# Chunked mLSTM followed by two feed-forward layers on one core: the state update moved ahead of the denominators, matmuls of ones added in the late units, and three steps of the later stages moved

## Chip, cores and metric

One core of one Trainium2 chip. The metric is the device time of one execution in microseconds (us), lower is better. The time before is the median of three runs; a profiled execution is told apart from them below.

## What is computed

Three layers, one after the other. B, H, S, D are 2, 8, 768, 40; the model width is H*D = 320 and there are 1536 tokens.

```python
# 1: per token t, state C (D x D) and n (D) of each head
m_new = max(f[t] + m, i[t]); f_stab = exp(f[t] + m - m_new); i_stab = exp(i[t] - m_new)
C = f_stab * C + i_stab * outer(v[t], k[t]);  n = f_stab * n + i_stab * k[t]
y[t] = sigmoid(o[t]) * (C @ q[t]) / max(abs(n . q[t]), 1)
# 2: four experts, all of them for every token
x = sum over e of p[:, e] * (relu(x @ w1[e]) @ w2[e])        # w1: 320 x 1024, w2: 1024 x 320
# 3: gated layer
out = ((x @ w_a) * (x @ w_b)) @ w_out                         # 320 x 1536, 1536 x 320
```

## The kernel before

**First layer, in units.** The sequence is cut into chunks of 128 tokens; a unit is one chunk of one batch, so there are NU = 12 units, and batch b of unit u is u % 2. For each unit TensorE (PE) makes the scores of queries and keys (`products`, L1245), the products with the incoming state (`from_state`, L1257), the products of weighted scores and values (`outputs`, L1286) and the addition to the state (`update`, L1271); `log_weights` (L1233, L1234) makes the decay weights of the next unit. The order on PE is written out by hand: in the loop over u come `log_weights(u + 1)`, `products(u)`, `from_state(u)`, in units 3 to 8 the turning of an earlier unit's finished output (`x_transpose`, four transposes, L1202 and L1204), `outputs(u - 1)` and `update(u - 1)`. `from_state(u)` waits for the state that `add_update(u - 2)` leaves.

VectorE (DVE) multiplies scores by weights (`weigh`, L896), scales the products with the state (`scale_inter`, L904), takes the numerators (`take_num`, L932), divides (`normalise`: three small instructions for the denominators, L940 to L944, and one for the quotient, L948), and adds to the state (`add_update`, L921), in this order. GpSimd (POOL) decays the state (L428), gates the output (`gate_output`, L441) and does parts of the weights: `sums` are four additions of 128 x 128 (L457 to L463), `low_a` and `low_s` the low halves of a split of the float32 weights in two (L447, L452). ScalarE (ACT) makes the high halves (`high_a` L633, `high_s` L637) and copies.

**Second and third layers, in groups.** The rest of the program is NG = 56 groups, of which the first FIRST = 32 belong to the experts and the others to the gated layer. A group makes two blocks of 128 hidden columns for half of the tokens by a scheme of seven products of half-size blocks instead of eight (`product(n, i)`, four matmuls each, L1358 to L1361, into two PSUM banks A and B in turn), and between them, in slots, the second layer of the group before (`second_layer`, L1382). How many of its matmuls go into each slot is the table `chunks(n)`. ACT copies three of the products out (`keep_p1` L675, `keep_u2` L681, `keep_w` L687); DVE adds to them (`make_c11` L1056, `make_c22` L1063, `make_c12` L1070) and makes the low halves of the hidden values (`low_relu` L1041, `low_product` L1047). Product 5 waits for `keep_w`, product 6 for `make_c22`, and the first product of the next group for the low half of the second hidden block (`a_free`).

The input of these groups is itself held as seven sums and differences of blocks: `x_sum` (four subtractions, on DVE L880 or on POOL L489), `x_high` (ACT L597) and `x_low` (DVE L870, L871). There are four such sets of input, numbered s = 0 to 3. Sets 1, 2 and 3 are turned by PE within groups 1 and 2, 29 and 30, 33 and 34 (`turning(n)`): three turns (`turn_within`) in each of these groups, each into bank B, each copied out by ACT (`keep_turn`, L582) before the bank is written again. `set_at(n, k)` is the set that stands k steps after its base in group n; so the x_sums of set 1 lie in groups 2 and 3, those of set 2 in groups 30 and 31, and in groups 4, 32 and 36 the products of a new set begin.

`keep_busy` (L1211) and `keep_warm` (L1217) are matmuls of constants whose results nobody reads; there are 32 of ones in units 0 and 1 and 13 of the identity in group 0.

Of the kernel before, what the change touches and what calls it, by code (L numbers as in the profile page):

```python
# [53 lines left out]
def mlstm_moe_kernel(nc, qk_t, tok, gates, late, probs, wt, wtail, w2, w_out, out):  # L54
    with ExitStack() as ctx:
# [156 lines left out]
            return 4 * min(n, FIRST) + 2 * max(n - FIRST, 0)  # L212

        BASES = {1: 0, 2: FIRST - NP1, 3: FIRST}
        TURN_AFTER = (0, 1, 2)

        def set_at(n, k):

# [34 lines left out]
        def chunks(n):  # L253

            if turning(n) is not None:
                return (3, 6, 5, 0, 3, 6, 1, 5, 4, 3) if n <= FIRST else (0, 3, 3, 0, 2, 3, 0, 3, 2, 2)
            if n == NG - 1:
                return (0, 2, 1, 1, 3, 3, 8)
            return (4, 5, 5, 5, 8, 5, 4) if n <= FIRST else (0, 3, 2, 2, 5, 4, 2)
# [130 lines left out]
        def _(pool):  # L390
# [101 lines left out]
            for u in range(NU):  # L492
                if B <= u < OLD:
                    decay_state(u)
                if u < OLD:
                    update_keys(u)
                if u >= 1:
                    sigmoid(u - 1)
                    gate_output(u - 1)
                if u == 3:  # L500
                    tails_low_a(0)
                if u == 4:
                    tails_sums(0)
                if u == 5:
                    tails_low_s(0)
                    low_a(0)
                if u == 6:
                    sums(0)
                if u == 7:
                    low_s(0)  # L510
                    low_a(1)
                if u == 8:
                    sums(1)
                if u in (8, 9, 10):
                    x_sum(0, u - 8)
                if u == 10:
                    x_sum(0, 3)
            sigmoid(NU - 1)
            low_s(1)
            gate_output(NU - 1)  # L520
            for i in range(2, NP1):
                low_a(i)
                sums(i)
# [1 line left out]
            for n in range(NG):  # L525
                st = n // (2 * NP1)
                if set_at(n, 3) == 3:
                    for j in range(1, 4):
                        x_sum(3, j)
                for i in range(NP1, NS * NP1):  # L530
                    if a_at(i) + 1 == n:
                        low_s(i)
                    if a_at(i) == n:
                        low_a(i)
                        sums(i)
                if n % (2 * NP1) == 4 and st + 1 < NS:
                    tails_low_a(st + 1)
                    tails_sums(st + 1)
                if n % (2 * NP1) == 5 and st + 1 < NS:
                    tails_low_s(st + 1)  # L540
                if set_at(n, 2) == 3:
                    x_sum(3, 0)


        @block.scalar
        def _(act):
# [174 lines left out]
            for u in range(1, NU):  # L721
                if u == 1:
                    gates_of(1)
                if u + 1 < NU:
                    weights(u + 1)
                if u == 1:
                    act.wait_ge(ex_turned, 2)
                    nc.scalar.activation(ex[:, :, :, :].rearrange("p a c h -> p (a c h)"), PS[:, XPOSE, BH:BH + 3 * REST], ACT.Exp).then_inc(ex_ready, 1)
                if u >= 2:
                    replicate((u - 2) // UB, (u - 2) % UB)  # L730
                if 0 <= u - 3 < UB:
                    keep_turned(0, u - 3, XPOSE)
                if u >= 2:
                    gates_of(u)
                if u == 2:
                    nc.scalar.dma_start(t1[:, :], wtail[0, :, :]).then_inc(t1_in, 16)
                if 2 <= u <= NP1 + 1:
                    load_first(u - 2)
                if 6 <= u <= 9:
                    load_first_w2(u - 6)  # L740
                if u == 3:
                    tails_high_a(0)
                if u == 4:
                    high_a(0)
                if u == 5:
                    tails_high_s(0)
                if u == 6:
                    high_a(1)
                if u == 7:
                    high_s(0)  # L750
                if u == 9:
                    high_s(1)
                if 6 <= u <= 10:
                    x_high(0, u - 6)
                if u in (9, 10):
                    high_w2(u - 9)
                if u == 11:
                    x_high(0, 5)
                    x_high(0, 6)
# [26 lines left out]
            def expert_group(n):  # L786
# [8 lines left out]
                if b2 is not None:  # L795
                    x_high(b2, 0)
                high_c11(n)
                keep_turn(n, 1)
                keep_u2(n)
                keep_turn(n, 2)  # L800
                if b2 is not None:
                    x_high(b2, 1)
                if b3 is not None:
                    x_high(b3, 3)
                prepare_weights(n)
                keep_w(n)
                replicate_late(b1, 3)
                if b2 is not None:
                    x_high(b2, 2)
# [11 lines left out]
            def gated_group(n):  # L821
# [11 lines left out]
                    high_product(n - 1, 1)  # L833
                if b2 is not None:
                    x_high(b2, 0)
                keep_turn(n, 1)
                keep_u2(n)
                keep_turn(n, 2)
                if b2 is not None:
                    x_high(b2, 1)  # L840
                if b3 is not None:
                    x_high(b3, 4)
                keep_w(n)
                replicate_late(b1, 3)
                if b2 is not None:
                    x_high(b2, 2)
                prepare_weights(n)
                if b3 is not None:
                    x_high(b3, 5)
# [13 lines left out]
        def _(dve):  # L863
# [158 lines left out]
            for u in range(NU):  # L1022
                if u == 0:
                    rest_logs()
                weigh(u)
                if u >= B:
                    scale_inter(u)
                if u >= 1:
                    take_num(u - 1)
                    normalise(u - 1)  # L1030
                    if u - 1 < OLD:
                        add_update(u - 1)
                if u >= 7:
                    x_low(0, u - 7)
                if u == 11:
                    low_w2(0)
# [73 lines left out]
            def expert_group(n):  # L1110
# [16 lines left out]
                if b3 is not None:  # L1127
                    x_low(b3, 3)
                    x_sum(b3, 1)
                    x_sum(b3, 2)  # L1130
                if b4 is not None:
                    x_low(b4, 5)
                    x_low(b4, 6)
                make_c22(n)
                if p == 0:
                    add_tiles(n, range(HB))
                w2_lows(n)
                low_relu(n, 1, PS[:, A_BANK, 0:HT])
                low_relu(n, 2, c22_s[:, :])
# [7 lines left out]
                    x_low(b2, 2)  # L1147
                    x_sum(b2, 0)
                if b3 is not None:
                    x_sum(b3, 3)  # L1150
                    x_low(b3, 4)

            def gated_group(n):
# [40 lines left out]
        def _(pe):  # L1194
# [228 lines left out]
            for u in range(1, NU):  # L1423
# [3 lines left out]
                if u == 1:  # L1427
                    keep_busy(3)
                    log_weights(2)
                if u >= B:  # L1430
                    from_state(u)
                if 0 <= u - 3 < UB:
# [6 lines left out]
            for n in range(NG):  # L1439
                slot = 0  # L1440
                for i in range(7):
                    product(n, i)
                    between(n, slot)
                    slot += 1
                    if turning(n) is not None and i in TURN_AFTER:
                        turn_within(n, TURN_AFTER.index(i))
                        between(n, slot)
                        slot += 1
            for j in range(3 * HB * tiles(NG - 1)):
# [37 lines left out]
```

## Time and profile before

| | us |
|---|---|
| median of three runs | 637.74 |
| lowest, highest | 635.42, 637.91 |
| the profiled execution | 639.25 |
| its span, first to last instruction | 637.5 |
| PE busy | 617.9 (97%) |
| VectorE, ScalarE, GpSimd busy | 374.3, 301.6, 217.1 |
| mean granted TensorE clock | 0.977 |

The units take the first 87.7 us of the span, group 0 the next 15.1, and the groups after it the rest. A float32 matmul of the units shows as two instructions in the trace. "Busy" of PE is from a matmul's start to its modelled end, so that a busy PE can still be at half its clock; the granted clock is a row of its own. The waits view puts idle time of an engine down to the instruction that ended it.

### The profile page before, as it was taken

Reading aid. Unit: us, or ns where it says so; the run is one execution under the profiler, and the core shown is the slowest. Engines: PE = TensorE matmul, PEld = TensorE weight load, DVE = VectorE, ACT = ScalarE, POOL = GpSimd, SP = SyncE. Lnnn points to the kernel's source line nnn. Section 1 sums busy time; section 2 is a strip of 40 time slices with the busy share of each in tenths; the row PEclk is TensorE's granted clock in tenths of the full one; section 3 lists DMA queues with packets and bytes.
Section 4 is the critical chain, followed back from the end, with each engine's and each line's share of the span. In section 5 each row is a group of like instructions: output and inputs, shape, how many; then the busy total and the mean of one; then the engine's idle time right before and its main releaser. Section 6 shows DMA issues by size and latency. Waiting matters only on the chain. (4 is left out here: it accounts for less than half of the span.)

```text
span 637.5 us, 11103 instructions
## 1 busy us (share of the span) xinstructions
PE 617.9 (97%) x4005; PEld 594.1 (93%) x4015; DVE 374.3 (59%) x716; ACT 301.6 (47%) x644; POOL 217.1 (34%) x285
## 2 busy tenths in 40 slices
PE   8999999999999999999999999998989999999997
PEld 7888798989999999999999999988879999999997
DVE  6667785676354444463534635377597564656565
ACT  3688734653444333543435434665554443444332
POOL 3378863304250033510243201254144640463000
PEclk9999659999999999999999999999999999999999
DMA  3657504100232002320014100112100420030011
GB/s 119 197 198 190 157 0 135 55 22 1 66 93 75 22 1 66 93 75 22 1 44 104 55 12 1 45 23 83 53 12 1 99 85 28 9 80 1 1 63 62
DMA packets 21062, 38.96 MB, mean 61 GB/s; under 512 B 3600, under 2 KB 11312, under 8 KB 21008
## 3 DMA queue, kind: packets, MB, share of 16 engines
q1 hardware_dynamic: 18976, 35.57, 19.8%
q10 hardware_dynamic: 2032, 2.68, 1.5%
q8 instruction: 32, 0.52, 0.3%
q14 instruction: 22, 0.18, 0.1%
HBM read 26.42 MB, written 1.97 MB: 45 GB/s over the span
## 5 line engine op out<-in xcount | busy, mean ns | idle before, releaser
L1382 PE MATMUL PS<-w2h,hh 128*128 128x320 f32 x528 | 164.3, 311 | 0.0
L1382 PE MATMUL PS<-w2h,hl 128*128 128x320 f32 x528 | 163.8, 310 | 0.0
L1382 PE MATMUL PS<-w2l,hh 128*128 128x320 f32 x528 | 163.3, 309 | 0.0
L1358 PE MATMUL PS<-xop,wop 128*128 128x384 f32 x392 | 139.9, 357 | 9.4 <-DVE c_s L1063 2.3
L669 ACT ACTIVATE hh<-c_s 128x384 fp32r<-128x384 f32 x144 | 75.3, 523 | 130.7 <-DVE c_s L1070 42.2
L1361 PE MATMUL PS<-xop,wop 96*128 96x384 f32 x392 | 132.9, 339 | 0.0
L1359 PE MATMUL PS<-xop,wop 128*128 128x384 f32 x392 | 132.6, 338 | 0.0
L1360 PE MATMUL PS<-xop,wop 128*128 128x384 f32 x392 | 132.5, 338 | 0.0
L1063 DVE TENSOR_TENSOR c_s<-PS,w_s 128x384 f32<-128x384 f32 x56 | 31.2, 557 | 124.1 <-ACT w_s L687 89.1
L1382 PEld LDWEIGHTS PS<-w2h,hh 128*128 128x128 f32 x528 | 99.6, 189 | 0.8 <-DVE hl L1047 0.7
L1382 PEld LDWEIGHTS PS<-w2l,hh 128*128 128x128 f32 x528 | 99.6, 189 | 0.0
L1382 PEld LDWEIGHTS PS<-w2h,hl 128*128 128x128 f32 x528 | 99.5, 188 | 0.0
L1358 PEld LDWEIGHTS PS<-xop,wop 128*128 128x128 f32 x392 | 74.1, 189 | 19.8 <-issue 4.0
L452 POOL TENSOR_TENSOR wop<-s,wop 128x512 fp32r<-128x512 f32 x28 | 37.2, 1327 | 136.4 <-ACT wop L637 136.4
L1041 DVE SCALAR_TENSOR_TENSOR hl<-c_s,hh 128x384 fp32r<-128x384 f32 x96 | 55.0, 572 | 41.9 <-ACT hh L669 41.7
L1359 PEld LDWEIGHTS PS<-xop,wop 128*128 128x128 f32 x392 | 74.3, 190 | 0.0
L1361 PEld LDWEIGHTS PS<-xop,wop 96*128 96x128 f32 x392 | 74.1, 189 | 0.0
L1360 PEld LDWEIGHTS PS<-xop,wop 128*128 128x128 f32 x392 | 74.1, 189 | 0.0
L687 ACT ACTIVATE w_s<-PS 128x384 f32<-128x384 f32 x56 | 27.5, 490 | 75.3 <-PE PS L1361 75.2
L471 POOL TENSOR_TENSOR t1l<-t,t1h 128x384 fp32r<-128x384 f32 x7 | 7.1, 1020 | 130.2 <-ACT t1h L643 130.2
L1056 DVE TENSOR_TENSOR c_s<-PS,p_s 128x384 f32<-128x384 f32 x56 | 31.0, 554 | 21.6 <-PE PS L1361 21.3
L447 POOL TENSOR_TENSOR wop<-s,wop 128x384 fp32r<-128x384 f32 x28 | 29.8, 1065 | 40.7 <-ACT wop L633 40.7
(137 smaller groups left out, 867.6 us busy)
## 6 DMA issues: line engine op xcount, KB each, us to landing
wop<-t1h SPq DMA_DIRECT2D x56, 112.0 KB, 2.2
s<-in_wt SPq DMA_DIRECT2D x24, 256.0 KB, 3.2
kvo<-in_tok SPq DMA_DIRECT2D x12, 480.0 KB, 4.3
qk<-in_qk_t SPq DMA_DIRECT2D x24, 160.0 KB
s<-in_w SPq DMA_DIRECT2D x12, 320.0 KB, 3.0
wop<-t1l SPq DMA_DIRECT2D x28, 112.0 KB, 2.2
s<-in_w_out SPq DMA_DIRECT2D x12, 160.0 KB, 2.2
out_y<-acc SPq DMA_DIRECT2D x12, 160.0 KB, 1.9
```

The costliest lines, as they stand in the source:

```text
L447: nc.gpsimd.tensor_tensor(wop[p][:, 2, 0:3 * P], s1[:, p, P:4 * P], f32(wop[p][:, 0, 0:3 * P]), ALU.subtract).then_inc(w_lo_a, 1)
L452: nc.gpsimd.tensor_tensor(wop[p][:, 2, 3 * P:7 * P], s1[:, p, :], f32(wop[p][:, 0, 3 * P:7 * P]), ALU.subtract).then_inc(w_lo_s, 1)
L669: nc.scalar.activation(hh[:, home(n, k), :], src, ACT.Relu if n < FIRST else ACT.Copy).then_inc(hh_ready, 1)
L687: nc.scalar.activation(w_s[:, :], PS[:, A_BANK, 0:HT], ACT.Copy).then_inc(w_kept, 1)
L1041: nc.vector.scalar_tensor_tensor(out=hl[:, home(n, k), :], in0=src, scalar=0.0, in1=f32(hh[:, home(n, k), :]), op0=ALU.max, op1=ALU.subtra ...
L1056: nc.vector.tensor_tensor(c11_s[:, :], PS[:, B_BANK, 0:HT], p1_s[:, :], ALU.add).then_inc(c11_made, 1)
L1063: nc.vector.tensor_tensor(c22_s[:, :], PS[:, B_BANK, 0:HT], w_s[:, :], ALU.add).then_inc(c22_made, 1)
L1358: nc.tensor.matmul(bank, ws[0], xs[0], start=opens, stop=False, skip_group_check=True)
L1359: nc.tensor.matmul(bank, ws[0], xs[2], start=False, stop=False, skip_group_check=True)
L1360: nc.tensor.matmul(bank, ws[2], xs[0], start=False, stop=False, skip_group_check=True)
L1361: nc.tensor.matmul(bank, ws[1][0:96, :], xs[1][0:96, :], start=False, stop=closes, skip_group_check=True).then_inc(prod_done, 1)
L1382: got = nc.tensor.matmul(bank, left, (w2l if part == 1 else w2h)[p][:, f, :], start=opens and part == 0, stop=closes and part == 2)
```

## The change

In the units, `add_update(u - 1)` stands ahead of `normalise(u - 1)` on DVE. In units 7 to 11 PE does three matmuls of ones between `products(u)` and `from_state(u)`, behind a wait for `scale_inter(u - 1)`, since they write into the same bank that it reads. The four additions `sums(1)` on POOL move from unit 8 to behind the units, ahead of the last `gate_output`; `high_s(1)` on ACT moves from unit 9 to group 0, ahead of `keep_w`, and the other weights that ACT prepares in group 0 move behind `keep_w`. In the turning groups the second and third turn stand behind the third product, instead of behind the second and the third, with other counts in the slots and with `keep_u2` ahead of the second copy. The third x_sum of sets 1 and 2 moves behind `make_c22`, their fourth from DVE to POOL. In group 35 `x_high` of step 4 moves behind `keep_w`.

```diff
-        TURN_AFTER = (0, 1, 2)
+        TURNS_AFTER = {0: (0,), 2: (1, 2)}
...
             if turning(n) is not None:
-                return (3, 6, 5, 0, 3, 6, 1, 5, 4, 3) if n <= FIRST else (0, 3, 3, 0, 2, 3, 0, 3, 2, 2)
+                return (3, 6, 1, 0, 6, 6, 1, 6, 4, 3) if n <= FIRST else (0, 5, 1, 0, 4, 4, 0, 3, 1, 0)
...
# POOL, units
-                if u == 8:
-                    sums(1)
...
             sigmoid(NU - 1)
+            sums(1)
+            gate_output(NU - 1)
             low_s(1)
-            gate_output(NU - 1)
...
# POOL, groups
+                if set_at(n, 3) in (1, 2):
+                    x_sum(set_at(n, 3), 3)
...
# ACT, units
-                if u == 9:
-                    high_s(1)
...
# ACT, expert_group
+                keep_u2(n)
                 keep_turn(n, 1)
-                keep_u2(n)
                 keep_turn(n, 2)
...
-                prepare_weights(n)
+                if n:
+                    prepare_weights(n)
+                else:
+                    high_s(1)
                 keep_w(n)
+                if n == 0:
+                    prepare_weights(n)
...
# ACT, gated_group
-                if b3 is not None:
-                    x_high(b3, 4)
                 keep_w(n)
                 replicate_late(b1, 3)
                 if b2 is not None:
                     x_high(b2, 2)
+                if b3 is not None:
+                    x_high(b3, 4)
...
# DVE, units
                     take_num(u - 1)
-                    normalise(u - 1)
                     if u - 1 < OLD:
                         add_update(u - 1)
+                    normalise(u - 1)
...
# DVE, expert_group
                     x_sum(b3, 1)
-                    x_sum(b3, 2)
...
                 make_c22(n)
                 if p == 0:
                     add_tiles(n, range(HB))
+                if b3 is not None:
+                    x_sum(b3, 2)
...
-                    x_sum(b3, 3)
                     x_low(b3, 4)
...
# PE
+                if u > UB:
+                    pe.wait_ge(inter_scaled, u - B)
+                    keep_busy(3)
                 if u >= B:
                     from_state(u)
...
-                    if turning(n) is not None and i in TURN_AFTER:
-                        turn_within(n, TURN_AFTER.index(i))
+                    for k in TURNS_AFTER.get(i, ()) if turning(n) is not None else ():
+                        turn_within(n, k)
```

The instructions of PE in unit 9 (scores, state, outputs, addition to the state), before:

```order
L1245 MATMUL PS<-qk 128x128 x8
L1257 MATMUL PS<-state,qk 128x82 x4
L1286 MATMUL PS<-vx,pt 128x41 x8
L1271 MATMUL PS<-vx,kw 40x41 x8
L1233 MATMUL PS<-mask,identb 128x512
```

And with the change (every line number of PE is four higher):

```order
L1249 MATMUL PS<-qk 128x128 x8
L1215 MATMUL PS<-ones 128x128 x3
L1261 MATMUL PS<-state,qk 128x82 x4
L1290 MATMUL PS<-vx,pt 128x41 x8
L1275 MATMUL PS<-vx,kw 40x41 x8
L1237 MATMUL PS<-mask,identb 128x512
```

The three matmuls of ones stand where PE had only the wait for the state. In the same unit on DVE, from the scaling of the products with the state to the quotient, before:

```order
L904 TENSOR_TENSOR inter_s<-PS,ex 128x328
L932 TENSOR_TENSOR num<-PS,inter_s 128x328
L940 SCALAR_TENSOR_TENSOR den<-num 128x8
L942 TENSOR_SCALAR den<-den 128x8
L944 RECIPROCAL den<-den 128x8
L948 TENSOR_TENSOR normed<-num,den 128x320
L921 TENSOR_TENSOR state<-PS,state 40x4x41 x2
```

With the change:

```order
L908 TENSOR_TENSOR inter_s<-PS,ex 128x328
L936 TENSOR_TENSOR num<-PS,inter_s 128x328
L925 TENSOR_TENSOR state<-PS,state 40x4x41 x2
L944 SCALAR_TENSOR_TENSOR den<-num 128x8
L946 TENSOR_SCALAR den<-den 128x8
L948 RECIPROCAL den<-den 128x8
L952 TENSOR_TENSOR normed<-num,den 128x320
```

The two additions to the state now run before four instructions that they don't need, and the quotient behind two more than before. On ACT, from the end of the last unit into group 0, before:

```order
L597 ACTIVATE xop<-raw 128x2x384 x2
L675 ACTIVATE p_s<-PS 128x384
L669 ACTIVATE hh<-c_s 128x384
L681 ACTIVATE u_s<-PS 128x384
L633 ACTIVATE wop<-s 128x384
L687 ACTIVATE w_s<-PS 128x384
L669 ACTIVATE hh<-PS 128x384
```

With the change:

```order
L598 ACTIVATE xop<-raw 128x2x384 x2
L676 ACTIVATE p_s<-PS 128x384
L670 ACTIVATE hh<-c_s 128x384
L682 ACTIVATE u_s<-PS 128x384
L638 ACTIVATE wop<-s 128x512
L688 ACTIVATE w_s<-PS 128x384
L634 ACTIVATE wop<-s 128x384
L670 ACTIVATE hh<-PS 128x384
```

The copy of the fifth product (w_s) no longer stands behind the high half of a weight that waits for the last gated output, but behind one that waits for the four additions of `sums(1)`.

## Rows read from the trace of the kernel before

**Rows 1.** Page, parts 1 and 2: busy time, and the granted clock in 40 slices.

```profile
PE 617.9 (97%) x4005; PEld 594.1 (93%) x4015; DVE 374.3 (59%) x716; ACT 301.6 (47%) x644; POOL 217.1 (34%) x285
...
PEclk9999659999999999999999999999999999999999
```

**Rows 2.** Waits of PE: waiting <- waited for: us in total, times, longest.

```profile
PE PS L1257 <- DVE state L921: 2.4, 4, 1.0
...
PE PS L1358 <- DVE xop L871: 2.2, 4, 0.8
...
PE PS L1358 <- ACT w_s L687: 1.7, 2, 1.3
```

**Rows 3.** Windows of 2 us: length, busy of each engine, then clock, DMA, GB/s.

```profile
66.00:68.00 2.00, 1.23 (x11) 1.23 (x12) 1.91 (x5) 0.90 (x4) 1.72 (x3) 1.00 0.98 272
68.00:70.00 2.00, 2.00 (x17) 1.92 (x16) 1.90 (x4) 2.00 (x6) 1.84 (x4) 0.77 0.58 181
...
86.00:88.00 2.00, 2.00 (x10) 2.00 (x11) 0.11 (x2) 0.76 (x2) 2.00 (x3) 0.50 0.00 0
...
96.00:98.00 2.00, 2.00 (x14) 2.00 (x14) 1.76 (x6) 0.31 (x1) 0.00 (x0) 0.91 0.00 0
```

**Rows 4.** Timeline, PE: from_state of units 7 to 11, first product of group 0.

```profile
53.70 1.12 PE L1257 MATMUL PS<-state,qk 128*128 128x82 f32 x8 [0.59 <-DVE state L921]
...
59.94 1.12 PE L1257 MATMUL PS<-state,qk 128*128 128x82 f32 x8 [0.42 <-DVE state L921]
...
66.77 1.12 PE L1257 MATMUL PS<-state,qk 128*128 128x82 f32 x8 [1.02 <-DVE state L921]
...
74.54 2.00 PE L1257 MATMUL PS<-state,qk 128*128 128x82 f32 x8
...
82.53 2.00 PE L1257 MATMUL PS<-state,qk 128*128 128x82 f32 x8
...
87.67 0.67 PE L1358 MATMUL PS<-xop,wop 128*128 128x384 f32 x1
```

**Rows 5.** Timeline, DVE, unit 9: numerators, quotient, state.

```profile
63.83 0.49 DVE L932 TENSOR_TENSOR num<-PS,inter_s 128x328 f32<-128x328 f32 x1
...
65.63 0.49 DVE L948 TENSOR_TENSOR normed<-num,den 128x320 f32<-128x320 f32 x1
66.04 0.68 DVE L921 TENSOR_TENSOR state<-PS,state 40x164 f32<-40x164 f32 x2
```

**Rows 6.** Timeline, PE, unit 1: three matmuls of ones and the next.

```profile
17.82 0.94 PE L1211 MATMUL PS<-ones 128*128 128x128 f32 x6
18.59 0.38 PE L1233 MATMUL PS<-mask,identb 128*128 128x512 bf16 x1
```

**Rows 7.** Timeline, PE: sixth product of group 0, first of group 1.

```profile
100.53 0.41 PE L1358 MATMUL PS<-xop,wop 128*128 128x384 f32 x1 [1.25 <-ACT w_s L687]
...
102.81 0.42 PE L1358 MATMUL PS<-xop,wop 128*128 128x384 f32 x1
```

**Rows 8.** Timeline, PE: last product of group 3, third of group 4.

```profile
136.89 0.44 PE L1358 MATMUL PS<-xop,wop 128*128 128x384 f32 x1 [0.34 <-DVE c_s L1063]
...
141.63 0.44 PE L1358 MATMUL PS<-xop,wop 128*128 128x384 f32 x1 [0.46 <-DVE xop L871]
```

**Rows 9.** Timeline, groups 31 and 32.

```profile
426.95 3.62 DVE L880 TENSOR_TENSOR raw<-raw 128x768 f32<-128x768 f32 x2
...
431.09 0.44 PE L1358 MATMUL PS<-xop,wop 128*128 128x384 f32 x1 [1.92 <-DVE c_s L1063]
...
431.36 0.54 DVE L1041 SCALAR_TENSOR_TENSOR hl<-PS,hh 128x384 fp32r<-128x384 f32 x1
...
432.49 0.34 PE L1358 MATMUL PS<-xop,wop 128*128 128x384 f32 x1
...
435.96 0.44 PE L1358 MATMUL PS<-xop,wop 128*128 128x384 f32 x1 [0.59 <-DVE xop L871]
```

**Rows 10.** Timeline, PE, group 33: second product, second turn, fourth product.

```profile
445.51 0.44 PE L1358 MATMUL PS<-xop,wop 128*128 128x384 f32 x1 [0.24 <-ACT raw L582]
...
447.13 0.33 PE L1202 MATMUL PS<-identf,acc 128*128 128x128 f32 x1 [0.21 <-DVE c_s L1056]
...
450.01 0.41 PE L1358 MATMUL PS<-xop,wop 128*128 128x384 f32 x1 [0.33 <-ACT raw L582]
```

More of the change, by code:

```diff
@@ L835, in gated_group @@
                     x_high(b2, 0)
+                keep_u2(n)
                 keep_turn(n, 1)
-                keep_u2(n)
                 keep_turn(n, 2)
```

## The prediction

> **What bounds the kernel now.** I read the page first. PE is busy for 617.9 of 637.5 us, so only two things can give much: its clock and its few waits. The row of the clock shows both levels: 9 (2.4 GHz) nearly everywhere, but 6 and 5 in the fifth and sixth of the 40 slices, from 64 to 96 us [rows 1]. The windows of 2 us place it: 1.00 up to 68 us, 0.77 in the next (half of the clock from about 69.1 on), 0.50 until 96, and 0.91 in the window at 96, so full again from about 96.4 [rows 3]. That is 27.3 us at 1.2 GHz, and PE is busy without a break in nearly all of it: there each microsecond of work at the full clock takes two.
>
> The timeline says where this lies: `from_state` of unit 9 begins at 66.77, after PE had been idle for 1.02 us; units 10 and 11 follow at 74.54 and 82.53, and group 0 begins at 87.67 [rows 4]. What did PE do before the clock fell? Units 7 and 8 had idle times of 0.59 and 0.42 us and four transposes each, and held the clock; unit 9 is the first with the longer idle and without transposes. The idle time ends each time with DVE's addition to the state. On DVE, numerators begin at 63.83, quotient at 65.63, state at 66.04 [rows 5]: 1.7 us of denominators and quotient stand between, which the state does not need.
>
> The waits view lists the rest: 2.4 us for the state, 2.2 for low halves of the input (x_low), 1.7 for w_s, of which 1.3 in group 0 [rows 2]. I looked at each in the timeline [rows 7 to 10].
>
> **The change part by part.** The sum is made against the profiled execution, 639.25 us (span 637.5); the median of the runs, 637.74, is 1.5 below it, which I take off at the end.
>
> *State ahead of the denominators.* The state comes about 1.7 us earlier behind the numerators. The waits of units 7, 8 and 9 (0.59, 0.42, 1.02) go, and one of 0.36 in unit 6 (2.4 less these, [rows 2]). Late next is the quotient, by the 0.68 us of the additions: behind it are the gated output on POOL, ACT's copy of it and the values for the next outputs. They are wanted a unit later, so I cost that at nothing; without that cover it would be 0.7 us a unit.
>
> *Ones.* Three matmuls took 17.82 to 18.59 at the full clock, 0.77 us [rows 6]. There are five units with them. In units 7 and 8 they cost 1.54, and with unit 6 the waits give back 1.37: together +0.2.
>
> *Units 9 to 11 and group 0, if the clock holds.* Unit 8 to unit 9 took 6.83 us at the full clock [rows 4]; without the 1.02 and with ones that is 6.58: -0.25. From unit 9 to 10 the transposes are gone too (0.4 or so): 6.2 for 7.77, -1.6. From unit 10 to 11, where no decay weights are left to make, 7.99 at half clock is 4.0 at full, 4.8 with ones. DVE can't follow that: its work of a unit fills most of 1.91 and 1.90 in windows of 2 us beside POOL [rows 3], so some 6 us a unit. I take 5.8: -2.2; the bounds are 4.8 and 6.6. From there to group 0: 5.14, half is 2.6: -2.5. Group 0 took 102.81 - 87.67 = 15.14 us. Of it 8.7 ran at half clock (87.67 to 96.4), 4.4 at full; the other 6.4 contain the wait of 1.25 for w_s [rows 7], which `keep_w` ahead of the weights removes. That leaves 9.5. But now DVE and ACT are late: DVE has x_low, low_w2 and the last numerators ahead of c11, and w_s stands behind `high_s(1)`, which waits for POOL to finish the last x_sums, two sigmoids and `sums(1)`. I put 1.6 on it (bounds 0.5 and 3): 11.1, so -4.0. These four come to **-10.6** (bounds -8 and -12.5).
>
> The Trainium skill (TensorE: Matmul & The Clock Gate, Part 1 and "Why this matters for your kernels") says the clock follows how busy PE was, and advises against idle gaps between matmuls. The rows agree with the gap before the fall, but not that busy time alone gives the clock back: the window at 86 us is full of PE work at 0.50. By that rule alone the ones would still do, since they fill the gap.
>
> *Groups 3 and 4.* The last product of group 3 waited 0.34 for c22 behind two x_sums; the third of group 4 waited 0.46 for x_low [rows 8], behind the fourth. One x_sum now runs behind c22, one on POOL. With the restart of the pipeline after each wait, -1.0.
>
> *Groups 31 and 32.* The wait is larger, 1.92 us, since two x_sums took 3.62 us beside POOL's work [rows 9]. But it does not all come back: group 32's first product must wait for hl, at 431.36 + 0.54 = 431.90, and DVE has the same work ahead of that as before. So 432.49 becomes 431.95 at best: -0.5. The 0.59 at the third product of group 32 shrinks as the fourth x_sum leaves DVE, though POOL then works beside it: -0.2. Together -0.7 (bounds 0 and -1.2).
>
> The Trainium skill (SBUF — State Buffer, "Who interferes with whom") says that a DVE instruction with two inputs in SBUF contends with a reading GpSimd one. By it a subtraction on POOL is not free to DVE: with the whole of it charged to DVE the last 0.2 would be a loss.
>
> *Turns behind the third product.* In group 33 the waits of 0.24, 0.21 and 0.33 [rows 10] recur in group 34. The second product now has five matmuls instead of three between the turn and itself, the second turn a whole product behind the one that c11 is made from, and the fourth product four matmuls instead of three. The waits of both groups are 1.56; I take 1.5, since a rest may stay but each wait also restarts the pipeline. In groups 1, 2, 29 and 30 the same gives 0.3 in all. New is the third turn's wait for ACT, which now has `keep_u2` before the second copy; six matmuls cover it in the expert groups, four barely in the gated ones. -1.8 (bounds -0.8 and -2.2).
>
> *Group 35.* The other wait for w_s (1.7 - 1.25, [rows 2]) goes, but x_low on DVE is late at group 36's third product anyway (the 0.8 of [rows 2]): 0.
>
> Sum: +0.2 - 10.6 - 1.0 - 0.7 - 1.8 = -13.9; 639.25 - 13.9 - 1.5 = 623.9. I say **624.3**, since DVE's part is the one I know least.
>
> **Rivals.** *The clock falls one unit later.* In units 9 and 10 state products, outputs and updates still follow each other without transposes, and ones only precede them. Then unit 10 to 11 takes 8.0 and 1.5 for ones, the rest as before except for the 1.25: 9.5 for 5.8, 5.1 for 2.6 and 13.9 for 11.1 make 9.0, and 624.3 + 9.0 = 633.3, less if the fall comes within unit 11. For it: the clock fell in just such a unit. Against: the idle time is gone, and ones are six passes where the transposes were four. Chance 0.17.
>
> *Ones don't count,* so that the clock falls as it did: the ones then cost 3.0 in units 10 and 11, and what is left of the gain is 3.5 in the groups and the 1.25: 637.7 + 3.0 - 4.75 = 636. Chance 0.07. The skill's page (TensorE: Matmul & The Clock Gate, Part 4) says transposes don't count as busy for the clock; by that the units with transposes held it in spite of waits of 0.59, and the idle of 1.02 alone made it fall, which speaks for the forecast.
>
> *The clock falls earlier: slower.* In units 7 and 8 ones are ahead of a state that may still be late, through a quotient that is 0.68 later on POOL and ACT. If PE then idles for over 1 us in unit 7, as it did in unit 9, units 7 and 8 take 8.0 us, as units 10 and 11 did, and 1.5 for ones, instead of the 6.3 of the full clock (6.24 from unit 7 to 8, [rows 4]), and units 9 to 11 each 1.5 more than before: 6.4 + 4.5, less 3.5 and 1.25 later, so 637.7 + 6.2 = 644. It decides from an idle of about 1 us. Against: that chain has a unit of slack. Chance 0.04.
>
> *The later edits give nothing,* since each wait reappears at the next product: 628, within the forecast's side. Chance 0.10.
>
> **How the numbers follow.** The forecast has 0.62. Its own range is 620.5 to 628; the later edits giving nothing (628) and the later fall (633.3) are taken in, and about 0.2 is left out: ones that don't count, the early fall, and the ends of the bounds. A measurement of this kernel tells about 0.5% (3.2 us, so 634.5) from no change. Faster: 0.62 + 0.10 + most of 0.17, 0.84. Same: the rest of it and ones that don't count, 0.11. Slower 0.05.
>
> **What would show it.** Granted clock 1.00 from the first units to the end, group 0 at about 81 us, group 1 at about 92. No wait for the state in units 6 to 11; DVE busy over 0.9 in the last units. No wait of over 0.6 us at the last product of group 31, but its next group starting only 0.5 earlier. Group 33 0.7 shorter. A clock row with 5 in it would make the prediction wrong, by 2 us for each unit and 4 for group 0.

## The result

| | before | after |
|---|---|---|
| median, us | 637.38 (6 runs) | 632.53 (6 runs) |
| lowest, highest | 635.42, 639.84 | 631.24, 633.46 |
| profiled execution, its span | 639.25, 637.5 | 632.11, 630.3 |
| PE, DVE, POOL busy | 617.9, 374.3, 217.1 | 614.3, 375.2, 221.6 |
| mean granted clock | 0.977 | 0.989 |

The ratio is 0.9921, 95% interval [0.9898, 0.9944]: faster by 0.8%, 4.9 us. The forecast was 13 us. Of the experiments below, one execution of s2_ones_alone (666.88 us, clock 0.846) and one of s3_group0_alone (752.45 us, clock 0.731) are left out of the ratios.

The page's row of the clock has one 6 in place of the 6 and 5 of [rows 1]:

```profile
PE 614.3 (97%) x4035; PEld 590.1 (94%) x4045; DVE 375.2 (60%) x714; ACT 300.2 (48%) x644; POOL 221.6 (35%) x289
...
PEclk9999959999999999999999999999999999999999
```

The windows of 2 us, where the columns are those of [rows 3]. The clock is full until about 81.1 us, half until about 94.7, full again after it: 13.7 us instead of 27.3.

```profile
80.00:82.00 2.00, 0.91 (x5) 0.94 (x5) 1.93 (x5) 1.73 (x4) 1.87 (x3) 0.77 0.00 0
...
86.00:88.00 2.00, 2.00 (x8) 1.96 (x8) 1.97 (x3) 0.00 (x0) 1.84 (x4) 0.50 0.00 0
...
94.00:96.00 2.00, 2.00 (x14) 2.00 (x13) 0.37 (x1) 0.51 (x3) 1.84 (x4) 0.82 0.74 171
```

The PE timeline answers to [rows 4] and [rows 7] (every PE line is four higher): the states of units 7 to 11, group 0 with its waits, the first product of group 1.

```profile
52.06 1.02 PE L1261 MATMUL PS<-state,qk 128*128 128x82 f32 x8
...
58.47 1.02 PE L1261 MATMUL PS<-state,qk 128*128 128x82 f32 x8
...
65.19 1.02 PE L1261 MATMUL PS<-state,qk 128*128 128x82 f32 x8
...
71.21 1.02 PE L1261 MATMUL PS<-state,qk 128*128 128x82 f32 x8
...
76.40 1.02 PE L1261 MATMUL PS<-state,qk 128*128 128x82 f32 x8
...
79.00 0.42 PE L1362 MATMUL PS<-xop,wop 128*128 128x384 f32 x1
...
81.09 1.90 PE L1290 MATMUL PS<-vx,pt 128*128 128x41 f32 x8 [1.13 <-DVE num L936]
...
89.00 0.66 PE L1362 MATMUL PS<-xop,wop 128*128 128x384 f32 x1 [0.75 <-DVE c_s L1060]
...
96.92 0.42 PE L1362 MATMUL PS<-xop,wop 128*128 128x384 f32 x1
```

No state is waited for any more, and the units run near the forecast or better: 6.72, 6.02, 5.19 and 2.60 us from unit 8 to group 0, where it said 6.58, 6.2, 5.8 and 2.6. But group 0 takes 17.92 us, where before took 15.14 and the forecast said 11.1. The reader sees why on DVE, in the same stretch:

```profile
78.73 1.29 DVE L900 TENSOR_TENSOR pt<-PS,wgt 128x512 f32<-128x512 f32 x2
79.94 0.49 DVE L908 TENSOR_TENSOR inter_s<-PS,ex 128x328 f32<-128x328 f32 x1
80.35 0.49 DVE L936 TENSOR_TENSOR num<-PS,inter_s 128x328 f32<-128x328 f32 x1
80.87 0.84 DVE L944 SCALAR_TENSOR_TENSOR den<-num 128x8 f32<-128x8 f32 x1
81.74 0.92 DVE L946 TENSOR_SCALAR den<-den 128x8 f32<-128x8 f32 x1
...
83.00 0.81 DVE L952 TENSOR_TENSOR normed<-num,den 128x320 f32<-128x320 f32 x1
...
85.44 1.37 DVE L890 TENSOR_TENSOR w2l<-s,w2h 128x640 fp32r<-128x640 f32 x1
...
88.30 0.56 DVE L1060 TENSOR_TENSOR c_s<-PS,p_s 128x384 f32<-128x384 f32 x1
...
90.68 0.17 DVE L944 SCALAR_TENSOR_TENSOR den<-num 128x8 f32<-128x8 f32 x1
90.89 0.17 DVE L946 TENSOR_SCALAR den<-den 128x8 f32<-128x8 f32 x1
```

DVE works without a gap up to 92.4: weighted scores, numerators, quotient, input halves, w2l, then at 88.30 c11, which PE waits for at 89.00. In the windows at 80 and 86 it is busy 1.93 and 1.97 of 2 us. Up to the product that needs c11, the fourth of the group, PE could be as fast as it liked.

The waits of PE, those of [rows 2] among them: the 2.4 for the state and the 1.7 for w_s are gone; waits for DVE's halves have come instead.

```profile
PE PS L1362 <- DVE xop L875: 3.1, 4, 1.5
...
PE PS L1362 <- DVE hl L1045: 1.4, 4, 0.9
PE PS L1362 <- DVE c_s L1060: 1.3, 2, 0.7
PE PS L1290 <- DVE num L936: 1.1, 1, 1.1
```

Lengths of the stages, between first products in the two traces:

| stage | before | after | forecast of the difference | measured |
|---|---|---|---|---|
| to from_state of unit 2 | 24.2 | 22.9 | 0 | -1.3 |
| from there to unit 8 | 35.7 | 35.5 | +0.2 | -0.15 |
| unit 8 to group 0 | 27.7 | 20.5 | -6.6 | -7.2 |
| group 0 | 15.14 | 17.92 | -4.0 | +2.8 |
| groups 1 to 4 | 47.02 | 46.08 | -1.15 | -0.9 |
| groups 5 to 28 | 245.6 | 245.6 | 0 | 0 |
| groups 29, 30 | 24.34 | 24.08 | -0.15 | -0.3 |
| groups 31, 32 | 23.78 | 24.17 | -0.7 | +0.4 |
| groups 33 to 36 | 39.77 | 39.33 | -1.5 | -0.4 |

The first row is not the change. It holds of the edits only the order of the state in unit 1, and in the profiles below it is 22.9 to 24.3 with the old order and 22.8 to 26.0 with the new one.

Groups 31 and 32, which answer to [rows 9]:

```profile
426.16 1.20 DVE L1045 SCALAR_TENSOR_TENSOR hl<-c_s,hh 128x384 fp32r<-128x384 f32 x1 [0.59 <-ACT hh L670]
427.28 1.35 DVE L874 TENSOR_TENSOR xop<-raw,xop 128x384 fp32r<-128x384 f32 x1
...
424.79 0.41 PE L1362 MATMUL PS<-xop,wop 128*128 128x384 f32 x1 [0.89 <-DVE hl L1045]
...
429.26 0.45 PE L1362 MATMUL PS<-xop,wop 128*128 128x384 f32 x1 [1.52 <-DVE xop L875]
...
425.92 2.30 POOL L489 TENSOR_TENSOR raw<-raw 128x384 f32<-128x384 f32 x2
```

The wait of 1.92 is gone, 0.89 of it is back at the next group's first product, as forecast, and the 0.59 has become 1.52: the fourth x_sum starts on POOL only behind its weight additions, and stretches DVE's two instructions to 1.20 and 1.35 (0.56 and 0.55 without it, in e4_xsum_dve below).

### The profile page after: what moved, and what is told of

Its sections match the earlier page's. It is cut to its first block and busy times, and to the rows that moved or that the text cites. A ratio compares the mean times of both kernels' runs of the same rounds, so it can differ in the third digit from the quotient of the medians.

```text
span 630.3 us, 11170 instructions
## 1 busy us (share of the span) xinstructions
PE 614.3 (97%) x4035; PEld 590.1 (94%) x4045; DVE 375.2 (60%) x714; ACT 300.2 (48%) x644; POOL 221.6 (35%) x289
## 3 DMA queue, kind: packets, MB, share of 16 engines
HBM read 26.42 MB, written 1.97 MB: 45 GB/s over the span
```

## Experiments

Three sets of kernels, each beside runs of before on the same chip (medians 637.17, 636.29 and 636.78).

| run | what | median, us | ratio to before |
|---|---|---|---|
| e1_warm | after, clock held longer | 632.65 | 0.9933 [0.9917, 0.9950] |
| e2_no_ones | after without ones | 631.32 | 0.9924 [0.9895, 0.9954] |
| e3_old_state | after, old order of the state | 633.15 | 0.9942 [0.9924, 0.9960] |
| e4_xsum_dve | after, fourth x_sum on DVE | 631.76 | 0.9927 [0.9907, 0.9946] |
| s1_state_alone | before + state ahead | 635.93 | 1.0004 [0.9981, 1.0027] |
| s2_ones_alone | before + ones | 636.28 | 0.9991 [0.9977, 1.0006] |
| s3_group0_alone | before + edits for w_s | 635.06 | 0.9976 [0.9957, 0.9995] |
| t1_later_alone | before + edits of groups 1 to 36 | 634.51 | 0.9974 [0.9959, 0.9990] |
| t3_old_turns | after, turns as before | 633.39 | 0.9949 [0.9928, 0.9969] |
| s4_lean | after, DVE relieved in group 0 | 630.71 | 0.9911 [0.9895, 0.9928] |
| t2_lean_no_ones | s4_lean without ones | 631.80 | 0.9930 [0.9906, 0.9954] |
| t4_lean_split | s4_lean, one x_sum on DVE | 630.29 | 0.9898 [0.9879, 0.9916] |

**Is it the clock that group 0 lacks?**

```diff
                 if n == 0:
+                    if slot == 0:
+                        pe.wait_ge(raw_ready, UB)
+                        for _ in range(6):
+                            nc.tensor.matmul(PS[:, XPOSE, 0:P], identf[:, :], identf[:, :], start=True, stop=True)
                     if slot < 2:
                         outputs(NU - 1, (slot,))
```

> The changed kernel with six matmuls of the identity into a free PSUM bank in group 0, after the first product and ahead of the outputs of the last unit, where PE idled for 1.13 us just before the clock fell at 81.1 us. Theory (that idle time, new with the change, makes the clock fall in group 0): granted clock 1.00 through group 0, which shrinks from 17.9 us to some 12 to 14, DVE being full there; total about 628, 4 to 5 below the changed kernel's 632.5. Rival (group 0 has too little work for PE anyway, since DVE is the bound, and the clock falls a little later): 631 to 633, clock at one half in some 4 of the windows of 2 us as before.

The clock did hold longer (half from 87.9 to 94.8 only, 6.8 us instead of 13.7), and group 0 took 17.37. PE's timeline:

```profile
80.20 0.42 PE L1362 MATMUL PS<-xop,wop 128*128 128x384 f32 x1
...
86.66 0.44 PE L1362 MATMUL PS<-xop,wop 128*128 128x384 f32 x1 [1.71 <-DVE xop L875]
...
90.21 0.66 PE L1362 MATMUL PS<-xop,wop 128*128 128x384 f32 x1 [2.08 <-DVE c_s L1060]
```

What the clock gave back stands as two waits for DVE, and my theory of 628 fell. The fourth product, which needs c11, starts 10.01 us after the first here and 10.00 in after: up to it DVE bounds group 0. The 0.55 that is saved lies behind it, where PE is at half clock until 94.8 in both.

What the clock is worth behind it shows e4_xsum_dve (below), which differs from after in later groups alone. There too the fourth product starts 10.00 us after the first (79.14), but the clock is full again from 92.3 on, and group 0 took 16.74:

```profile
89.14 0.66 PE L1361 MATMUL PS<-xop,wop 128*128 128x384 f32 x1 [1.05 <-DVE c_s L1058]
...
95.88 0.42 PE L1361 MATMUL PS<-xop,wop 128*128 128x384 f32 x1
```

That is 6.74 us behind the fourth product, where after has 7.92. So group 0 is DVE's up to c11, and PE's, at the clock that it gets, behind it.

**Relieve DVE.** The low half of w2 (1.37 us) leaves its place ahead of c11, and c11 goes ahead of a further input half:

```diff
-                if u == 11:
-                    low_w2(0)
...
-                if n == 0:
-                    x_low(0, 5)
                 make_c11(n)
                 if n == 0:
+                    x_low(0, 5)
                     x_low(0, 6)
                     take_num(NU - 1)
                     normalise(NU - 1)
                 low_relu(n, 0, c11_s[:, :])
+                if n == 0:
+                    low_w2(0)
```

> The changed kernel with DVE relieved ahead of group 0's c11: the low half of the first second-layer weights (1.37 us) behind the first low half of the hidden values, where DVE waits 1.45 us for w_s, and c11 ahead of x_low of step 5 (1.4 us). Theory (group 0 is bounded by DVE, whose c11 is late at 88.3 us, not by PE's clock): c11 some 2.5 us earlier, group 0 some 15 instead of 17.9, total 629.5 to 630.5. Rival (the length of group 0 is set by PE at half clock): 632 to 632.5.

```profile
78.86 0.42 PE L1361 MATMUL PS<-xop,wop 128*128 128x384 f32 x1
...
80.96 1.06 PE L1289 MATMUL PS<-vx,pt 128*128 128x41 f32 x8 [1.14 <-DVE num L936]
...
85.33 0.69 PE L1361 MATMUL PS<-xop,wop 128*128 128x384 f32 x1 [1.63 <-DVE xop L875]
...
85.30 0.56 DVE L1058 TENSOR_TENSOR c_s<-PS,p_s 128x384 f32<-128x384 f32 x1
...
94.01 0.42 PE L1361 MATMUL PS<-xop,wop 128*128 128x384 f32 x1
```

Group 0 took 15.15 instead of 17.92; groups 1 and 2 gave 0.8 of it back (24.93 for 24.11). So 2.0 us in the trace; by the ratios it is 0.6, with intervals that overlap. Not all of the 2.77 in group 0 is the order. c11 comes 6.4 us after the first product instead of 9.3, where the theory said 2.5 earlier, and the fourth product 8.62 after the first instead of 10.00, without a wait: 1.4 us. The other 1.4 lies behind it, where the clock was full again from 90.2 on (half from 83.4); e4_xsum_dve shows that it can come back sooner without this edit. Beside e1_warm, which has 6.8 us of half clock too, the fourth product comes 1.4 earlier after the first as well.

**The ones.** Taken out of after:

```diff
-                if u > UB:
-                    pe.wait_ge(inter_scaled, u - B)
-                    keep_busy(3)
                 if u >= B:
                     from_state(u)
```

> The changed kernel without the ones in units 7 to 11. Theory (the state ahead of the denominators alone removes the idle time, but units 9 and 10 without transposes lose the clock without the ones): the clock falls in unit 9 or 10, 1.5 to 3 us slower than the changed kernel, 634 to 636. Rival (removing the idle time was enough, ones are padding): the clock falls at the same place in group 0 or a little earlier, units 7 and 8 are 0.7 us shorter each, total 630.5 to 632.5.

The clock fell at 74.6 instead of 81.1. But the time is no longer: 631.32. The units took 81.26 us, 2.3 more, and group 0 only 14.43, 3.5 less. Of that 1.9 is before the fourth product, which starts at 89.37 without a wait, 0.4 later than in after: what PE loses before DVE's queue it need not wait for behind it. The other 1.6 lies behind it, with the clock full again from 91.6 on; whether the earlier fall brought that is open. Put into before alone, the same three lines with a +:

> The kernel before with one edit: ones in units 7 to 11. Theory (they hold the clock through unit 9 even behind the old order, but cost 0.77 us in each unit where PE is the bound, and the time won in units 10 and 11 is bounded by DVE): units 3 to 5 us shorter, group 0 1 to 3 longer, total 635 to 637. Rival (the wait for the state stays over 1 us and the clock falls in unit 9 as before, with the ones at half clock on top): 639 to 641.

Half clock only from 89.0 to 95.9, and still no gain; the price stands at c11 again. (In t1_later_alone, whose units are those of before and take 1.7 us more, the same product starts at 91.53, without a wait.)

```profile
81.69 0.42 PE L1358 MATMUL PS<-xop,wop 128*128 128x384 f32 x1
...
91.48 0.66 PE L1358 MATMUL PS<-xop,wop 128*128 128x384 f32 x1 [2.79 <-DVE c_s L1056]
```

And taken out of s4_lean, the same diff again:

> s4_lean without the matmuls of ones. Theory A (ones bring nothing, here as in e2): as fast as s4_lean or up to 1 us faster, 629.7 to 630.9. Theory B (they bring nothing in after only because DVE bounds the late units and group 0; with DVE relieved the held clock pays): slower than s4_lean by 1 us or more, 631.7 or over. The clock should fall at about 70 to 76 us, and group 0 start at about 81.

631.80 is 1.1 over s4_lean, on the side of theory B, but the two were measured on different chips and their intervals overlap: it suggests that the ones begin to pay once DVE is relieved, and doesn't show it. What they do to the clock is plainer: its mean is 0.984 to 0.989 in the six executions of this kernel, and 0.991 to 0.995 in the five of s4_lean.

**The state.** The old order in after:

```diff
+                    normalise(u - 1)
                     if u - 1 < OLD:
                         add_update(u - 1)
-                    normalise(u - 1)
```

> The changed kernel with the denominators and the quotient ahead of the state again. Theory (the ones hold the clock, the order of DVE saves some 1.4 us of waits in units 6 to 9): the waits for the state come back in part, the clock holds to group 0, 0.5 to 2 us slower than the changed kernel, 633 to 634.5. Rival (the idle time of over 1 us in unit 9 comes back and the clock falls there): 636 to 638.

633.15, with an interval that overlaps that of after. The first products of groups 0 and 1 are at 82.0 and 98.3 instead of 79.0 and 96.9, but the start was 1.4 slower in this profile: 1.7 us are lost by group 0, 0.8 of them are left at the fourth product, which waits for c11, and none at group 1. The new order alone, the reverse of this diff, on before:

> The kernel before with one edit: the state is added ahead of the denominators. Theory (DVE bounds the last units and group 0, so what shortens its way to the state gives only the idle time of units 6 to 9, and the clock falls all the same since the transposes end): the units 1.5 to 3 us shorter, clock at one half from unit 9 or 10 until 90 to 96 us, total 634.5 to 636. Rival (the idle time was what made the clock fall): clock held to group 0, 630 to 632.5.

No gain: the waits for the state go, and 0.85 for a transfer of queries and keys and 2.39 for the weighted scores come in their place. The profiled execution is one of the slower ones of its kernel (639.62), so only the kind of the waits is read from it.

```profile
65.69 1.16 PE L1245 MATMUL PS<-qk 64*128 64x128 f32 x16 [0.85 <-DMA qk<-in_qk_t]
...
78.08 2.08 PE L1245 MATMUL PS<-qk 64*128 64x128 f32 x16 [2.39 <-DVE pt L896]
```

**The edits for w_s,** on before:

```diff
-                if u == 8:
-                    sums(1)
...
             sigmoid(NU - 1)
+            sums(1)
+            gate_output(NU - 1)
             low_s(1)
-            gate_output(NU - 1)
...
-                if u == 9:
-                    high_s(1)
...
-                prepare_weights(n)
+                if n:
+                    prepare_weights(n)
+                else:
+                    high_s(1)
                 keep_w(n)
+                if n == 0:
+                    prepare_weights(n)
```

> The kernel before with the edits around group 0 alone: the four sums of the second weight pair behind the units on POOL, their high half in group 0, the fifth product's copy ahead of the other weights. Theory (POOL's work in unit 8 and 9 delayed nobody on the path; the wait of 1.25 us for w_s goes, but part of it comes back as the wait for the sums): group 0 0.5 to 1.2 us shorter, total 636 to 636.7. Rival (POOL's sums shared DVE's way to memory in units 8 and 9, and DVE gains there as well): 634.5 to 636, unit 9 shorter and its idle time under 0.7.

The ratio makes it 1.5 us, between 0.3 and 2.7. Group 0 took 14.82 after units of 81.97.

**The later groups.** The remaining edits on before: all of the change's diff but its parts for the units and group 0. Its lines:

```diff
+        TURNS_AFTER = {0: (0,), 2: (1, 2)}
...
+                if set_at(n, 3) in (1, 2):
+                    x_sum(set_at(n, 3), 3)
...
+                keep_u2(n)
                 keep_turn(n, 1)
-                keep_u2(n)
```

> The kernel before with the edits of the groups 1 to 36 alone (turns, slot counts, keep_u2 order, the x_sums and x_high of step 4); the units and group 0 are as before. The prediction put 3.5 us on these edits (1.0, 0.7 and 1.8): ratio to before 0.9945. My theory by now, from the lengths of the groups in the trace of after: groups 1-2 -0.2, 3-4 -0.7, 29-30 -0.3, 31-32 +0.4, 33-36 -0.4, together -1.2 us, ratio 0.998; each of these five lengths should be within 0.1 us of that in after's trace (24.1, 22.0, 24.1, 24.2, 39.3).

Ratio 0.9974, 1.7 us [0.6, 2.6]: the lengths of the five stages are those of after within 0.1 us, so 1.2 us is what they hold, and 3.5 is outside the interval. This kernel has the units of before, instruction for instruction, and its profile shows what the one of before didn't:

```profile
65.42 1.12 PE L1259 MATMUL PS<-state,qk 128*128 128x82 f32 x8 [0.89 <-DVE state L923]
71.87 1.12 PE L1259 MATMUL PS<-state,qk 128*128 128x82 f32 x8 [1.04 <-DVE state L923]
78.85 1.43 PE L1259 MATMUL PS<-state,qk 128*128 128x82 f32 x8 [2.05 <-DVE state L923]
83.42 0.67 PE L1360 MATMUL PS<-xop,wop 128*128 128x384 f32 x1
...
98.82 0.42 PE L1360 MATMUL PS<-xop,wop 128*128 128x384 f32 x1
```

The clock was full up to about 79.5 us, through an idle time of 0.89 in unit 9 and of 1.04 in unit 10, and group 1 begins at 98.82 instead of 102.81 (1.3 us of it from the start). s3_group0_alone, with the same order on PE and DVE in the units, shows the same: idle for 1.02 in unit 9, fall at 79.5.

**The turns.** After with the old places and counts, and `keep_u2` behind the second copy:

```diff
-        TURNS_AFTER = {0: (0,), 2: (1, 2)}
+        TURNS_AFTER = {0: (0,), 1: (1,), 2: (2,)}
...
-                return (3, 6, 1, 0, 6, 6, 1, 6, 4, 3) if n <= FIRST else (0, 5, 1, 0, 4, 4, 0, 3, 1, 0)
+                return (3, 6, 5, 0, 3, 6, 1, 5, 4, 3) if n <= FIRST else (0, 3, 3, 0, 2, 3, 0, 3, 2, 2)
```

> The changed kernel with the old places of the turns, the old slot counts and keep_turn(1) ahead of keep_u2. By the prediction the turns are worth 1.8 us: 634.3. By the trace of after they are worth 0.9 (24.3 for 24.1 in groups 1-2 and 29-30, 39.8 for 39.3 in 33-36): 633.4. Groups 33 and 34 should be 10.8 and 10.9 us long again, and 36 shorter than now.

633.39, and in the trace the turns are worth 0.9: 0.2 in groups 1 and 2, 0.25 in 29 and 30, 0.46 in 33 to 36. The wait that remains in 33 in after (34 has the same, 0.19), and the one of group 36 behind them, which is 0.81 with the old turns as well:

```profile
443.24 0.41 PE L1362 MATMUL PS<-xop,wop 128*128 128x384 f32 x1 [0.20 <-ACT raw L583]
...
470.06 0.44 PE L1362 MATMUL PS<-xop,wop 128*128 128x384 f32 x1 [0.81 <-DVE xop L875]
```

**The fourth x_sum.** Back to DVE for both sets in after:

```diff
-                if set_at(n, 3) in (1, 2):
-                    x_sum(set_at(n, 3), 3)
...
                 if b3 is not None:
+                    x_sum(b3, 3)
                     x_low(b3, 4)
```

> The changed kernel with the fourth x_sum of sets 1 and 2 on DVE again, where it stood before; the third stays behind make_c22. Theory (on POOL it starts late, behind the weight sums, and shares DVE's way to memory, so that x_low of groups 31 and 32 takes 1.20 and 1.35 us instead of 0.55 and the third product of group 32 waits 1.68 us): that wait shrinks to some 0.7, group 4 gains 0.1 or nothing, total 0.7 to 1.2 below the changed kernel, 631.5. Rival (the wait is that of DVE's own work, which then is longer by 0.95): no change, 632.5.

Groups 31 and 32 took 23.71 instead of 24.17, groups 3 and 4 22.26 instead of 21.97. So the x_sum on POOL helps in set 1 and hurts in set 2. DVE has the subtraction itself here (0.95), but its neighbours are short:

```profile
425.82 0.56 DVE L1043 SCALAR_TENSOR_TENSOR hl<-c_s,hh 128x384 fp32r<-128x384 f32 x1 [0.59 <-ACT hh L668]
426.29 0.95 DVE L882 TENSOR_TENSOR raw<-raw 128x768 f32<-128x768 f32 x1
427.16 0.55 DVE L872 TENSOR_TENSOR xop<-raw,xop 128x384 fp32r<-128x384 f32 x1
```

s4_lean with each set on its better engine, that is with `== 1` for `in (1, 2)` on POOL and `if b3 == 2` on DVE:

> s4_lean with the fourth x_sum of set 2 back on DVE, that of set 1 still on POOL. Theory: groups 31-32 take 23.7 us instead of 24.2 (as in e4) and groups 3-4 stay at 22.0 (e4 had 22.3): 630.2, the fastest of all versions. Rival: the difference of 0.5 in e4 was not from this edit; then 630.7 and 24.2 again.

630.29, ratio 0.9898 [0.9879, 0.9916]: groups 31 and 32 at 23.71, groups 3 and 4 at 21.97. It has the lowest median and ratio of all versions. That is 1.5 us under after by the ratios, whose intervals still overlap, so what the runs show surely is its 1.0% over before.

## Why the prediction was wrong

The sign held, and so did the mechanism in the units; the mechanism in group 0 and the size did not.

*Units, right.* Forecast -0.25, -1.6, -2.2 and -2.5 from unit 8 to group 0, sum -6.6; measured -7.2 in the trace. The ones held the clock, the state came in time. DVE followed at 5.2 us from unit 10 to 11 where I had put 5.8.

*Group 0, the step that failed.* "8.7 ran at half clock, 4.4 at full" took PE for the bound. It gave DVE and ACT 1.6 us of lateness "in bounds of 0.5 and 3"; the trace gives 17.92 - 9.5 = 8.4. An estimate splits it: in before the fourth product starts 8.11 us after the first, all of it at half clock, so at full clock some 4.1; it started 10.00 after, 5.9 late, and that is DVE's queue (e1_warm, s4_lean). The other 2.5 are half clock behind it, which the forecast had excluded. The missed point: DVE has the same queue in front of c11 however early PE arrives. In before [rows 3] it had 0.11 us of work in the window at 86; that slack was what the forecast spent twice, once to speed up the units and once for group 0. The trace of before has the queue, from the numerators of unit 10 to c11:

```profile
87.91 0.50 DVE L932 TENSOR_TENSOR num<-PS,inter_s 128x328 f32<-128x328 f32 x1 [1.89 <-PE PS L1286]
...
94.81 0.56 DVE L1056 TENSOR_TENSOR c_s<-PS,p_s 128x384 f32<-128x384 f32 x1
```

These are 6.9 us (7.95 in after), the numerators begin no sooner than the group, and c11's product starts 0.7 behind c11 in after: 7.6 against 4.1, an estimate of at least 3.5 of lateness, most of it from the trace of before. The forecast put 1.6 on it, with 3 as the bound. The error is 6.8 us: as much as lies between the -13.9 of the sum and the -7.2 of the spans, since what else failed (2.2 in the later groups) was balanced by the start and the units.

*Profiled against median, a term too small.* I took 1.5 off. But the profiled execution of before is one of those with a low mean clock: of 57 other executions of before, 11 show a mean clock under 0.98 (638.1 to 640.2 us, median 638.7), and 37 one of 0.984 to 0.987 (median 636.2). From 0.977 to 0.985 there are 0.008 x 637.5 x 2, about 10 us less at half clock, for 2.5 us of time. So most executions had less to win than the 27.3 us of [rows 1], and of 10 us of clock only a quarter came out as time. It is a tendency: the five executions at 0.980 took 636.1 to 637.6 too. These clocks were measured with the experiments; before the result there was the one of the profiled execution, with three times beside it that were all shorter.

*Cause of the fall, not confirmed.* I tied it to the idle time of 1.02 in unit 9 without transposes. Two profiles with the same units hold the clock through 0.89 to 1.04 there and let it fall some 10 us later, at 79.5, after idle times of 1.56 and 2.05. The Trainium skill (TensorE: Matmul & The Clock Gate, Part 1) says, of a kernel's start, that the point at which the clock changes varies from run to run of one kernel; the 69.1 and the 79.5 are falls within a kernel, of which that sentence does not speak, and vary likewise. Why it fell where it did stays open. The fall varies within one kernel's code too: after, t3_old_turns and e4_xsum_dve are the same up to group 0, and have half clock from 81.1 to 94.7, 81.4 to 95.1 and 82.1 to 92.3.

*w_s, right in kind.* Its wait of 1.25 went; alone the edit gave 1.5 us, as much as the wait, though in after it stands beside waits for DVE.

*Groups 3 and 4.* -1.0 forecast; -0.7 in the trace.

*Groups 31 and 32.* -0.7 forecast, +0.4 measured. The return of the wait at group 32's first product came as said, but not the -0.5 that was to be left of it: e4_xsum_dve, which has only the third x_sum moved in these groups, took 23.71, where before took 23.78. The -0.2 for POOL's x_sum was a loss of 0.5 (e4_xsum_dve), of the sign that the prediction gave for the case that all of POOL's work is charged to DVE: the Trainium skill (SBUF — State Buffer, "Who interferes with whom") was the better guide than the rows that I weighed it against, and the 1.20 and 1.35 above agree with it.

*Turns.* -1.8 forecast, -0.9 shown: groups 33 and 34 gained 0.77, of the waits of 1.56; ACT's copies are still 0.2 late, and 0.3 is given back in group 35 (9.07 us in after, 8.76 in t3_old_turns). Group 36 takes 9.3 with either turns, 9.07 in before: there the wait for w_s that group 35 lost is paid back, as the forecast's 0 for group 35 said.

*Rivals.* None of them came. The later fall of the clock was priced at 633.3, near the 632.5 measured, but it put the fall into unit 10 or 11 and the clock held through both: that it is near is luck. The one that was missing is DVE as the bound of group 0, though the forecast named DVE's part as the one least known.

The parts measured alone (-0.3 for the state, 0.6 for the ones, 1.5 and 1.7) make 3.5 by their ratios, and the whole 5.0 by its own; with intervals of 1 us and more on each, nothing shows that they need each other.

## What to carry to other kernels

Before a half clock is priced at twice the time, lay the next engine's queue beside it: where it has no slack, the clock is worth nothing up to the instruction that waits for it (10.00 us with half clock and 10.01 without), and the order of its instructions is the edit to make (w2l and one input half behind c11 brought the product that needs it 1.4 us forward). Behind that instruction the clock counts again (7.92 us or 6.74). An engine's idle time can be spent once. And before a long gap of one profiled execution becomes the largest term, see from the other executions' mean clock how usual it is.

## What the runs showed of the hardware

DVE's smallest instructions suffer most beside POOL. The two of 128 x 8 took 0.17 us each with POOL idle (90.68) and 0.84 and 0.92 beside its four subtractions (80.87), which are on POOL's row as

```profile
78.25 4.38 POOL L489 TENSOR_TENSOR raw<-raw 128x384 f32<-128x384 f32 x4
```

that is 1.1 us each: every one of them seems to have waited for most of one of these. One of the two has a single input. Instructions with an input in PSUM beside them kept their time (0.49 at 79.94 and 80.35). From 80.87 to 90.1 this stretching adds some 2.9 us to DVE's queue, by the durations that the same instructions have elsewhere.

PE busy nearly without a gap at half clock doesn't bring the full clock back soon: in after it stayed at half from 81.1 to 94.7, with one wait of 0.75 us once the outputs had begun at 81.09. With six more matmuls in the first slot of group 0 (e1_warm) the fall was at 87.9 and the end at 94.8. These are single profiles, and executions of the same code differ by up to 1.0 us in the fall and 2.8 in the return (above), so that the six matmuls left the end where it was is not shown.
